# Later folded weights and a reordered start in a retention + gated-MLP kernel on one core

## The chip, the cores and the metric

The kernel runs on one core of one Trainium2 chip. The metric is the device time of one execution in microseconds (us). Before the change three runs took 1231.11, 1231.14 and 1233.21 us, a median of 1231.14 us.

## The reference, cut to what matters

```python
# q, k, v: (8, 8, 576, 64): batch, heads, positions, head size; all float32
scores = q @ k.T / sqrt(64)                      # per batch and head
ret = scores * gamma[h] ** (i - j)  (i >= j, else 0)
x = (ret @ v)  -> 4608 tokens x 512
h = max(x @ w1, x @ w2, x @ w3)                  # 512 -> 768
x = h @ w_out                                    # 768 -> 512
a = x @ u1; b = x @ u2                           # 512 -> 1024
out = ((a * b) @ u3) @ u_out                     # 1024 -> 1024 -> 512
```

Since nothing stands between `u3` and `u_out`, the kernel computes their product WC = u3 @ u_out once (the folded weights) and applies it in the last stage.

## The kernel before, in words

The program has two parts. The first, some 174 us long, is the attention with decay; the second, some 1055 us, is four stages of dense products over 12 x 384 tokens. The change touches the first part only.

**Steps.** There are 32 pairs (batch, two heads), n = 0 to 31. A loop on every engine runs over m = 0 to 16 (`STEPS` = 17). In step m the pairs `made_in(m)` = 2m, 2m+1 are begun and `read_in(m)` = 2m-2, 2m-1 are finished. TensorE (PE) does per pair: `scores(n)` (keys times queries, L1120 and L1125), `sum_state(n)` (keys times decayed values, L1140: the state that later chunks see), `query_state(n)` (L1158) and `values(n)` (L1170). VectorE (DVE) multiplies the scores by the decay (`decay_scores`, L952, `decay_tail`, L961) and chains the states (`make_state`, L974 and L977). ScalarE (ACT) makes the decayed values (`decay_values`, L793) and copies results out (`read_values`, L804 and L809). GpSimd (POOL) makes the decayed queries (`decay_queries`, L674).

**Who waits for whom.** `scores(n)` writes the PSUM banks of pair n-2 and waits for all decays of the two pairs before (`decayed`), and for `x_out` of pair n-4. `query_state(n)` waits for the states of n and for the decays of the two pairs made in the step. `decay_scores(n)` on DVE comes in its order after `make_state` of the step before. `sum_state(n)` waits for the decayed values, for the keys (`k_loaded`) and for the states of the two pairs before.

**Order inside a step on PE:** scores, then quarters of WC, then query_state, sum_state, values. For the pairs in `SUMS_FIRST` = (4, 5), that is in step 2, the sums come before query_state.

**Folded weights.** WC is made of 8 blocks kb of 4 quarters; a quarter is 6 products of 512 columns (L1185, L1187, L1189). `u3` is loaded in 8 blocks into 2 buffers, split by ACT (`split_u3`, L820) and POOL (L674) into a high and a low part; `uo` in 4 parts, split by ACT (L814) and POOL or DVE. The quarters begin in step `WC_FROM` = 3: one in step 3, three in step 4 (two of them at the step's end, `late_quarters`), two in each of the steps 5 to 14, four in steps 15 and 16.

**Start.** PE begins with products on zeros (`run_idle`, L1197), in all 9+4+3+2+2 = 20. `query_powers` and `decay_powers` (L1204, L1211) build the decay tables; `qtab` is copied by ACT (L857) after `decay_values(0)`.

**Queues.** All data is loaded by SyncE (SP), on one DMA queue, in program order: `load_qk` (queries and keys of a pair, 128 x 1152 floats, 576 KB), `load_v` and `load_k` (256 KB each), `load_tails` (64 KB), `load_decay` (128 KB), `load_uo` and `load_u3` (512 KB each). From n = 6 `load_qk(n)` waits for `q_decayed` n-3 and `load_k(n)` for `state_summed` n-1, and what stands behind such a wait in SP's order waits too.

Of the kernel before, what the change touches and what calls it, by code (L numbers as in the profile page):

```python
# [4 lines left out]
P = 128  # L5
# [5 lines left out]
FT2 = F2 // P  # L11
# [4 lines left out]
NC = SEQ // CH  # L16
# [170 lines left out]
STEPS = NP // 2 + 1  # L187
WC_FROM = 3
QUARTERS = 4 * FT2

SUMS_FIRST = (4, 5)

# [9 lines left out]
def quarters(m):  # L204
    if m == WC_FROM:
        return range(1)
    if m == WC_FROM + 1:
        return range(1, 2)
    if m >= STEPS - 2:
        return range(QUARTERS - 4 * (STEPS - m), QUARTERS - 4 * (STEPS - m) + 4)  # L210
    return range(2 * (m - WC_FROM), 2 * (m - WC_FROM) + 2) if m >= WC_FROM else ()


def late_quarters(m):
    return range(2, 4) if m == WC_FROM + 1 else ()

# [10 lines left out]
def keys_sem(n):  # L227
    return 2 + n if n < 4 else n % 2


def keys_count(n):
    return 16 if n < 4 else 16 * ((n - 4) // 2 + 1)

# [10 lines left out]

U3_LOAD = {min(2 * kb + WC_FROM - 2, STEPS - 3): kb for kb in range(FT2)}
U3_SPLIT = {min(2 * kb + WC_FROM - 1, STEPS - 2): kb for kb in range(FT2)}
UO_SPLIT = {2: 0, 3: 1}
WC_READ = {min(2 * kb + WC_FROM + 1, STEPS - FT2 + kb): kb for kb in range(FT2)}
# [18 lines left out]
def build(nc, qk, vv, vt, kk, wB, wC, wI, u3T, uo, decay, powers, columns, outT):  # L267
# [11 lines left out]
    with ctx:  # L279
# [61 lines left out]
        ks = [at(f"ks{i}", [P, K_COLS], f32, (v_at + 6 * V_COLS * 4, o)[i]) for i in range(2)]  # L341
        ks_first = [at(f"ks_first{i}", [P, K_COLS], f32, 26112 + i * K_COLS * 4) for i in range(4)]
        qks_first = [at(f"qks_first{i}", [P, KQ_COLS], f32, 34304 + i * KQ_COLS * 4) for i in range(2)]
        o += K_COLS * 4
# [24 lines left out]
        def sem(name):  # L369
            return ctx.enter_context(nc.semaphore(name))  # L370
# [5 lines left out]
        vt_loaded = [sem(f"vt_loaded{i}") for i in range(3)]  # L376
        k_loaded = [sem(f"k_loaded{i}") for i in range(6)]
        dec_loaded = [sem(f"dec_loaded{i}") for i in range(2)]
# [55 lines left out]
        def keys_of(n):  # L434
            return ks_first[n] if n < 4 else ks[n % 2]

# [8 lines left out]
        def _(sp):  # L445
# [21 lines left out]
            def load_k(n):  # L467
                if n >= 6:
                    sp.wait_ge(state_summed, n - 1)
                sp.dma_start(keys_of(n)[:, :], kk[n, :, :]).then_inc(k_loaded[keys_sem(n)], 16)  # L470
# [89 lines left out]
            sp.dma_start(pows[0:HEADS, :], powers).then_inc(pows_loaded, 16)  # L560
            sp.dma_start(cols[:, :], columns).then_inc(cols_loaded, 16)
            load_v(0)
            load_k(0)
            load_qk(1)
            load_decay(1)
            load_v(1)
            load_k(1)
            load_qk(2)
            load_qk(3)
            load_v(2)  # L570
            load_v(3)
            load_k(2)
            load_k(3)
            load_tails(0)
            load_qk(4)
# [5 lines left out]
            for m in range(1, STEPS):  # L581
                if m == 1:
                    load_u3(0)
                    load_uo(0)
                if m == 2:
                    for n in made_in(3):
                        load_k(n)
                if m > 1 and m in U3_LOAD:
                    load_u3(U3_LOAD[m])
                if m in P1_W_LOAD:  # L590
                    load_weight(P1_W_LOAD[m])
                if m >= 4:
                    for n in made_in(m + 1):
                        load_k(n)
                for n in made_in(m + 2):
                    load_qk(n)
                for n in read_in(m):
                    if n >= PAIRS:
                        store_x(n)
                if 2 * m + 4 < NP:  # L600
                    load_two_v(m + 2)
                if m == 2:
                    load_uo(2)
                    load_uo(3)
                    for n in made_in(4):
                        load_k(n)
                if m == 1:
                    load_tails(2)
                    load_uo(1)
                if 2 * m + 4 < NP:  # L610
                    load_tails(m + 2)
                if m in WC_READ:
                    store_wc(WC_READ[m])
# [58 lines left out]
        def _(pool):  # L672
# [80 lines left out]
            nc.gpsimd.memset(pows[:, :], 0.0).then_inc(pows_zeroed, 1)  # L753
            for m in range(STEPS - 1):
                if m in U3_SPLIT:
                    split_u3(U3_SPLIT[m])
                for n in made_in(m):
                    decay_queries(n)
                if m == 3:
                    split_uo(1)  # L760
                    split_uo(2)
                    split_uo(3)
                if m in P1_W_SUM:
                    sum_weight(*P1_W_SUM[m])
                if m in P1_T:
                    combine(0, P1_T[m])
# [16 lines left out]
        def _(act):  # L783
# [72 lines left out]
            act.wait_ge(qtab_powers, 1)  # L856
            nc.scalar.copy(qtab[:, :], ps[:, 2, :]).then_inc(qtab_made, 1)  # L857
            decay_values(1)
            for m in range(STEPS):
                if m == 2:  # L860
                    split_u3(U3_SPLIT[m])
                if m in UO_SPLIT:
                    split_uo(UO_SPLIT[m])
                if m in U3_SPLIT and m != 2:
                    split_u3(U3_SPLIT[m])
                if m in WC_READ and not late_quarters(m):
                    read_wc(WC_READ[m])
                for n in read_in(m):
                    read_values(n)
                if m == 3:  # L870
                    split_uo(2)
                for n in made_in(m + 1):
                    decay_values(n)
                if m == 3:
                    split_uo(3)
                if m in WC_READ and late_quarters(m):
                    read_wc(WC_READ[m])
                if m in P1_W_HI:
                    split_weight(P1_W_HI[m], 0)
                    split_weight(P1_W_HI[m], 1)  # L880
                if m in P1_HI:
                    split_tokens(0, P1_HI[m])
# [55 lines left out]
        def _(dve):  # L938
# [50 lines left out]

            def split_uo(i):  # L990
                dve.wait_ge(uo_hi, i + 1)
                low(uolo[:, 2 * i:2 * i + 2, :], uoraw[:, 2 * i:2 * i + 2, :], uohi[:, 2 * i:2 * i + 2, :]
                    ).then_inc(uo_lo[i], 1)

            def split_weight(wi, part):
# [17 lines left out]
            for m in range(STEPS):  # L1013
                for n in made_in(m):
                    decay_scores(n)
                    if n == 0:
                        mask_decay()
                        make_state(n)
                for n in made_in(m):
# [5 lines left out]
                for n in made_in(m):  # L1025
                    if n:
                        make_state(n)
                if m == 2:
                    split_uo(0)

# [76 lines left out]
        def _(pe):  # L1107
            def scores(n):
                pe.wait_ge(qk_loaded[rows_sem(n)], rows_count(n))
                if n >= 2:  # L1110
                    pe.wait_ge(decayed, 3 * (n - n % 2))
                if n == 1:
                    pe.wait_ge(qtab_made, 1)
                if n >= 4:
# [95 lines left out]
            def query_powers():  # L1210
                nc.tensor.matmul(ps[:, 2, :], pows[:, 2 * P:3 * P], pows[:, 3 * P:], start=True, stop=True,  # L1211
                                 skip_group_check=True).then_inc(qtab_powers, 1)

            pe.wait_ge(idle_zeroed, 1)
            run_idle(9, S_WC)
            pe.wait_ge(zeroed, 10)
            for m in range(STEPS):
                for n in made_in(m):
                    scores(n)
                    if n == 0:  # L1220
                        pe.wait_ge(pows_loaded, 16)
                        decay_powers()
                        query_powers()
                        run_idle(4, 3)
                        sum_state(0)
                        run_idle(3, 3)
                    if n == 1:
                        pe.wait_ge(dec_made, 1)
                        run_idle(2, S_WC)
                        pe.wait_ge(state_made, NC)  # L1230
                        sum_state(1)
                        run_idle(2, S_WC)
                for i in quarters(m):
# [4 lines left out]
                for n in read_in(m):  # L1238
                    query_state(n)
                for n in made_in(m) if m else ():  # L1240
# [4 lines left out]
                for i in late_quarters(m):  # L1245
                    wc_quarter(i)

# [115 lines left out]
```

## Time and profile before

| | |
|---|---|
| median of 3 runs | 1231.14 us |
| the profiled execution, its own time | 1231.38 us |
| its span | 1229.5 us |
| PE busy | 1222.1 us, 99% |
| DVE, ACT, POOL busy | 737.7, 485.7, 433.3 us |
| granted TensorE clock | 1.0 |
| DMA queue, share of 16 engines over the span | 39.1% |

Busy time is the time in which an instruction of the engine runs; the span goes from the first to the last instruction. With PE at 99% the time can only change by what PE executes and by where it waits. The steps of the first part can be told in the PE timeline by the two groups of `scores`.

### The profile page before, as it was taken

What the parts mean: (1) busy time and instruction counts of PE and PEld (TensorE: products, weight loads), DVE (VectorE), ACT (ScalarE), POOL (GpSimd) and SP (SyncE); (2) the same over time, 40 slices, a digit from 0 to 9 for tenths busy, and PEclk for the clock granted to TensorE, in tenths of its full rate; (3) what the DMA queues carried; (4) which work ended last, traced back from release to release, by engine and by line L of the source; (5) the groups of instructions that cost most, each with busy time, mean ns of one, the idle gap of its engine ahead of it and who ended that gap; (6) DMA issues with size and microseconds to landing.
All of it is one profiled execution on the core that took longest, in us unless ns stands there. A gap on an engine that the chain in (4) does not pass through costs nothing. (4 is left out here: it accounts for less than half of the span.)

```text
span 1229.5 us, 21665 instructions
## 1 busy us (share of the span) xinstructions
PE 1222.1 (99%) x8594; PEld 1202.2 (98%) x8594; DVE 737.7 (60%) x1065; ACT 485.7 (40%) x781; POOL 433.3 (35%) x234
## 2 busy tenths in 40 slices
PE   9999999999999999999999999999999999999999
PEld 8899999999999999999999999999999999999998
DVE  6444648845545464668886777454545466786653
ACT  3433544523232232326655544242323234554441
POOL 3535528220201102053867761202020217366550
PEclk9999999999999999999999999999999999999999
DMA  9999934121203021054464441313131342444441
GB/s 346 337 337 353 336 125 146 52 78 38 92 26 104 26 70 60 34 173 144 152 228 171 160 157 52 104 52 110 52 116 53 109 179 96 154 155 161 159 157 65
DMA packets 87332, 169.55 MB, mean 138 GB/s; under 512 B 9272, under 2 KB 58680, under 8 KB 87232
## 3 DMA queue, kind: packets, MB, share of 16 engines
q1 hardware_dynamic: 87232, 168.17, 39.1%
q8 instruction: 68, 1.11, 0.4%
q14 instruction: 32, 0.26, 0.1%
HBM read 106.27 MB, written 61.87 MB: 137 GB/s over the span
## 5 line engine op out<-in xcount | busy, mean ns | idle before, releaser
L1261 PE MATMUL ps<-chi,whi 128*128 128x384 f32 x2016 | 674.4, 335 | 1.9 <-ACT w L931 0.7
L1263 PE MATMUL ps<-chi,wlo 128*128 128x384 f32 x2016 | 673.5, 334 | 0.0
L1262 PE MATMUL ps<-clo,whi 128*128 128x384 f32 x2016 | 673.4, 334 | 0.0
L674 POOL TENSOR_TENSOR raw<-raw,raw 128x768 f32<-128x768 f32 (+3 forms) x102 | 268.1, 2650 | 582.8 <-DMA raw<-xd 203.5
L1261 PEld LDWEIGHTS ps<-chi,whi 128*128 128x128 f32 x2016 | 378.4, 188 | 4.5 <-ACT w L931 1.4
L1262 PEld LDWEIGHTS ps<-clo,whi 128*128 128x128 f32 x2016 | 378.4, 188 | 0.0
L1263 PEld LDWEIGHTS ps<-chi,wlo 128*128 128x128 f32 x2016 | 378.4, 188 | 0.0
L940 DVE TENSOR_TENSOR clo<-raw,chi 128x768 fp32r<-128x768 f32 (+2 forms) x168 | 253.5, 1537 | 41.7 <-ACT chi L851 41.7
L851 ACT CAST chi<-raw 128x768 fp32r<-128x768 f32 (+2 forms) x168 | 180.1, 1081 | 90.5 <-PE ps L1263 48.1
L931 ACT COPY w<-ps 128x384 f32<-128x384 f32 x126 | 60.5, 480 | 238.4 <-PE ps L1263 237.0
L918 ACT COPY u<-ps 128x384 f32<-128x384 f32 x126 | 60.7, 482 | 160.5 <-PE ps L1263 158.9
L1074 DVE TENSOR_TENSOR h<-ps,u 128x384 f32<-128x384 f32 x66 | 36.6, 555 | 122.8 <-PE ps L1263 121.2
L1048 DVE TENSOR_TENSOR h<-ps,w 128x384 f32<-128x384 f32 x66 | 36.6, 555 | 93.3 <-PE ps L1263 87.2
L1048 DVE TENSOR_TENSOR w<-ps,w 128x384 f32<-128x384 f32 x60 | 33.4, 557 | 87.0 <-PE ps L1263 86.9
L897 ACT COPY s<-ps 128x384 f32<-128x384 f32 x126 | 60.6, 481 | 55.5 <-PE ps L1263 55.5
L910 ACT COPY h<-ps 128x384 f32<-128x384 f32 x66 | 31.6, 479 | 82.4 <-PE ps L1263 79.8
L1074 DVE TENSOR_TENSOR u<-ps,u 128x384 f32<-128x384 f32 x60 | 33.3, 555 | 49.6 <-PE ps L1263 49.6
L674 POOL TENSOR_TENSOR wraw<-w,wraw 128x256 f32<-128x256 f32 (+2 forms) x21 | 26.2, 1247 | 95.2 <-DMA w<-wC 67.8
L940 DVE TENSOR_TENSOR wlo<-wraw,whi 128x768 fp32r<-128x768 f32 (+4 forms) x42 | 57.9, 1390 | 2.8 <-POOL wraw L674 2.7
L674 POOL TENSOR_TENSOR qdec<-qks,qtab 128x512 f32<-128x512 f32 x30 | 38.5, 1306 | 41.9 <-PE ps L1158 41.9
L952 DVE TENSOR_TENSOR probs<-ps,dec 128x512 f32<-128x512 f32 x64 | 39.9, 683 | 22.1 <-PE ps L1125 22.1
L674 POOL TENSOR_TENSOR wraw<-wraw 128x256 f32<-128x256 f32 (+2 forms) x42 | 47.4, 1129 | 1.6
(61 smaller groups left out, 820.7 us busy)
## 6 DMA issues: line engine op xcount, KB each, us to landing
gd<-h SPq DMA_DIRECT2D x96, 192.0 KB, 1.9
raw<-gd SPq DMA_DIRECT2D x24, 768.0 KB, 6.3
qks<-qk SPq DMA_DIRECT2D x30, 576.0 KB, 7.3
hd<-h SPq DMA_DIRECT2D x72, 192.0 KB, 1.9
raw<-hd SPq DMA_DIRECT2D x24, 576.0 KB, 6.6
x2d<-h SPq DMA_DIRECT2D x48, 192.0 KB, 2.9
raw<-x2d SPq DMA_DIRECT2D x24, 384.0 KB, 4.5
outT<-h SPq DMA_DIRECT2D x48, 192.0 KB, 1.9
```

The lines of the kernel that those rows point to most:

```text
L674: return nc.gpsimd.tensor_tensor(out_, a, b, op)
L851: nc.scalar.copy(chi[st][pos][:, :, :], raw_block(tau, pos)[:, :, :]).then_inc(c_hi, 1)
L897: nc.scalar.copy(sbuf_s[it % 2][:, :], ps[:, X[it % 2], 0:N]).then_inc(s_made, 1)
L918: nc.scalar.copy(sbuf_u[it % 2][:, :], ps[:, X[it % 2], 0:N]).then_inc(u_made, 1)
L931: nc.scalar.copy(sbuf_w[it % 2][:, :], ps[:, X[it % 2], 0:N]).then_inc(w_made, 1)
L940: return nc.vector.tensor_tensor(out_, whole, hi.bitcast(f32), ALU.subtract)
L952: nc.vector.tensor_tensor(probs[n % 4][:, h, 0:NC * CH].rearrange("p (n c) -> p n c", c=CH), ps[:, 2 * (n % 2) + h, :].rearrange("p (n c) ...
L1048: nc.vector.tensor_tensor(to[:, :], ps[:, Z[g % 2], 0:N], sbuf_w[g % 2][:, :], ALU.add).then_inc(sum22, 1)
L1074: nc.vector.tensor_tensor(to[:, :], ps[:, Z[g % 2], 0:N], sbuf_u[g % 2][:, :], ALU.add).then_inc(sum12, 1)
L1261: nc.tensor.matmul(to, w1, x1, start=(start and k == 0), stop=False, skip_group_check=True)
L1262: nc.tensor.matmul(to, w1, x2, start=False, stop=False, skip_group_check=True)
L1263: last = nc.tensor.matmul(to, w2, x1, start=False, stop=(k == KH[st] - 1), skip_group_check=True)
```

## The change

The folded weights start in step 5: two quarters in each of the steps 5 to 12, four (a whole block) in steps 13 to 16. `late_quarters` goes. The loads and splits of `u3` and `uo` move with them: the first `u3` is loaded in step 3 and not in step 1, `uo` in steps 1 to 4, and in steps 11 to 14 the load of `u3` stands at the end of SP's step. Two more key buffers let keys 4 and 5 have places of their own, so that keys 6 and 7 are loaded in step 1 with no wait. `SUMS_FIRST` now holds 4 to 9, so the sums come first in steps 2, 3 and 4. On PE the first two steps are written out in another order, with 13 products on zeros, and SP loads the queries and keys of pair 1 ahead of the values and keys of pair 0.

```diff
-WC_FROM = 3
+WC_FROM = 5
+WC_WHOLE = 13
-SUMS_FIRST = (4, 5)
+SUMS_FIRST = (4, 5, 6, 7, 8, 9)
 def quarters(m):
-    if m == WC_FROM:
-        return range(1)
-    if m == WC_FROM + 1:
-        return range(1, 2)
-    if m >= STEPS - 2:
+    if m >= WC_WHOLE:
         return range(QUARTERS - 4 * (STEPS - m), QUARTERS - 4 * (STEPS - m) + 4)
-def late_quarters(m):
-    return range(2, 4) if m == WC_FROM + 1 else ()
-U3_LOAD = {min(2 * kb + WC_FROM - 2, STEPS - 3): kb for kb in range(FT2)}
-U3_SPLIT = {min(2 * kb + WC_FROM - 1, STEPS - 2): kb for kb in range(FT2)}
-UO_SPLIT = {2: 0, 3: 1}
+WC_STEP = [min(2 * kb + WC_FROM, STEPS - FT2 + kb) for kb in range(FT2)]
+U3_LOAD = {WC_STEP[kb] - 2: kb for kb in range(FT2)}
+U3_SPLIT = {WC_STEP[kb] - 1: kb for kb in range(FT2)}
+UO_LOAD = {1: (0,), 2: (1,), 3: (2,), 4: (3,)}
+UO_SPLIT = {3: (0,), 4: (1,), 5: (2, 3)}
...
 # SP, the first loads
+            load_qk(1)
+            load_decay(1)
             load_v(0)
             load_k(0)
-            load_qk(1)
-            load_decay(1)
+            load_qk(2)
+            load_qk(3)
             load_v(1)
             load_k(1)
-            load_qk(2)
-            load_qk(3)
...
 # SP, the loop
                 if m == 1:
-                    load_u3(0)
-                    load_uo(0)
-                if m == 2:
-                    for n in made_in(3):
-                        load_k(n)
-                if m > 1 and m in U3_LOAD:
+                    load_k(6)
+                    load_k(7)
+                for i in UO_LOAD.get(m, ()) if m > 1 else ():
+                    load_uo(i)
+                if m in U3_LOAD and m < WC_WHOLE - 2:
                     load_u3(U3_LOAD[m])
-                if m >= 4:
+                if m >= 3:
                     for n in made_in(m + 1):
                         load_k(n)
...
                 if m == 1:
                     load_tails(2)
-                    load_uo(1)
+                    load_uo(0)
                 if 2 * m + 4 < NP:
                     load_tails(m + 2)
+                if m in U3_LOAD and m >= WC_WHOLE - 2:
+                    load_u3(U3_LOAD[m])
...
 # DVE, the states of pairs 0 and 1
-                        make_state(n)
+                        make_state(0)
+                    if n == 3:
+                        make_state(1)
...
 # PE, the start
-            run_idle(9, S_WC)
+            run_idle(8, S_WC)
             pe.wait_ge(zeroed, 10)
+            scores(0)
+            pe.wait_ge(pows_loaded, 16)
+            decay_powers()
+            query_powers()
+            scores(1)
+            pe.wait_ge(dec_made, 1)
+            run_idle(1, S_WC)
+            pe.wait_ge(qtab_made, 1)
+            sum_state(0)
+            run_idle(4, S_WC)
+            scores(2)
+            scores(3)
+            query_state(0)
+            pe.wait_ge(state_made, NC)
+            sum_state(1)
+            values(0)
+            query_state(1)
+            values(1)
+            sum_state(2)
+            sum_state(3)
+            for m in range(2, STEPS):
```

## Rows read from the trace of the kernel before

**Rows 1.** The page: PE's busy time, and DMA busy in tenths of 40 slices.
```profile
PE 1222.1 (99%) x8594; PEld 1202.2 (98%) x8594; DVE 737.7 (60%) x1065; ACT 485.7 (40%) x781; POOL 433.3 (35%) x234
DMA  9999934121203021054464441313131342444441
```
**Rows 2.** Timeline of PE, the start: start us, length us, line, records, wait before.
```profile
1.06 4.10 PE L1197 MATMUL ps<-idle 128*128 128x128 f32 x18 [1.06 <-DVE idle L1007]
...
8.20 1.05 PE L1197 MATMUL ps<-idle 128*128 128x128 f32 x8
9.19 0.69 PE L1140 MATMUL ps<-vdec,ks_first 128*64 128x64 f32 x16
...
14.01 1.16 PE L1120 MATMUL ps<-qks 64*128 64x128 f32 x16
...
16.82 0.99 PE L1158 MATMUL ps<-qdec,state 64*64 64x128 f32 x16 [0.35 <-DVE probs L952]
```
**Rows 3.** Timeline of ACT, the start.
```profile
6.37 0.91 ACT L793 ACTIVATE vdec<-vs,cols 128x256 f32<-128x256 f32 x2 [4.15 <-DMA vs<-vv]
8.40 0.59 ACT L857 COPY qtab<-ps 128x512 f32<-128x512 f32 x1 [1.13 <-PE ps L1211]
```
**Rows 4.** Timeline of DVE, the start.
```profile
9.92 0.22 DVE L974 COPY state<-ps 128x64 f32<-128x64 f32 x1 [1.51 <-PE ps L1140]
10.18 0.91 DVE L977 SCALAR_TENSOR_TENSOR state<-state,cols,ps 128x64 f32<-128x64 f32 x3
12.04 1.29 DVE L952 TENSOR_TENSOR probs<-ps,dec 128x512 f32<-128x512 f32 x2 [0.95 <-PE ps L1125]
13.36 0.50 DVE L961 TENSOR_TENSOR probs<-ps,dec 64x128 f32<-64x128 f32 x2
```
**Rows 5.** One DMA each, issue and landing: values 0, queries 1, keys 8.
```profile
L453 SPq DMA_DIRECT2D vs<-vv x1: 427/427/427, 2.5 to 2.5; - x1
DMA to landing us min/median/max: 3.9/3.9/3.9
...
L450 SPq DMA_DIRECT2D qks_first<-qk x1: 441/441/441, 3.4 to 3.4; - x1
DMA to landing us min/median/max: 5.7/5.7/5.7
...
L470 SPq DMA_DIRECT2D ks<-kk x1: 328/328/328, 35.6 to 35.6; - x1
DMA to landing us min/median/max: 7.1/7.1/7.1
```
**Rows 6.** Timeline of PE: begin of steps 2, 3, 4, 5, 6, and inside 2 and 4.
```profile
21.99 1.16 PE L1120 MATMUL ps<-qks 64*128 64x128 f32 x16
...
24.37 1.15 PE L1140 MATMUL ps<-vdec,ks 128*64 128x64 f32 x32
25.45 1.76 PE L1158 MATMUL ps<-qdec,state 64*64 64x128 f32 x32
...
29.27 1.16 PE L1120 MATMUL ps<-qks 64*128 64x128 f32 x16
...
37.98 1.16 PE L1120 MATMUL ps<-qks 64*128 64x128 f32 x16
...
40.88 0.49 PE L1120 MATMUL ps<-qks 64*128 64x128 f32 x4 [0.84 <-issue]
...
50.79 1.16 PE L1120 MATMUL ps<-qks 64*128 64x128 f32 x16
...
60.88 1.16 PE L1120 MATMUL ps<-qks 64*128 64x128 f32 x16
```
**Rows 7.** Loads of u3 (median to landing); its last split on ACT and POOL.
```profile
u3raw<-u3T SPq DMA_DIRECT2D x8, 512.0 KB, 6.6
...
154.62 1.05 ACT L820 CAST u3hi<-u3raw 128x1024 fp32r<-128x1024 f32 x1
...
155.75 2.39 POOL L674 TENSOR_TENSOR u3lo<-u3raw,u3hi 128x1024 fp32r<-128x1024 f32 x1 [3.24 <-ACT u3hi L820]
```

More of the change, by code:

```diff
@@ L227, in keys_sem @@
 def keys_sem(n):
-    return 2 + n if n < 4 else n % 2
+    return 2 + n if n < 6 else n % 2
 def keys_count(n):
-    return 16 if n < 4 else 16 * ((n - 4) // 2 + 1)
+    return 16 if n < 6 else 16 * ((n - 6) // 2 + 1)
 def v_sem(n):
@@ L342, in build @@
         ks_first = [at(f"ks_first{i}", [P, K_COLS], f32, 26112 + i * K_COLS * 4) for i in range(4)]
+        ks_first += [at(f"ks_first{i}", [P, K_COLS], f32, 36864 + i * K_COLS * 4) for i in (4, 5)]
         qks_first = [at(f"qks_first{i}", [P, KQ_COLS], f32, 34304 + i * KQ_COLS * 4) for i in range(2)]
@@ L376, in build @@
         vt_loaded = [sem(f"vt_loaded{i}") for i in range(3)]
-        k_loaded = [sem(f"k_loaded{i}") for i in range(6)]
+        k_loaded = [sem(f"k_loaded{i}") for i in range(8)]
         dec_loaded = [sem(f"dec_loaded{i}") for i in range(2)]
@@ L434, in keys_of @@
         def keys_of(n):
-            return ks_first[n] if n < 4 else ks[n % 2]
+            return ks_first[n] if n < 6 else ks[n % 2]
         def rows_of(n):
@@ L467, in load_k @@
             def load_k(n):
-                if n >= 6:
+                if n >= 8:
                     sp.wait_ge(state_summed, n - 1)
@@ L561, in _ @@
             sp.dma_start(cols[:, :], columns).then_inc(cols_loaded, 16)
+            load_qk(1)
+            load_decay(1)
             load_v(0)
             load_k(0)
-            load_qk(1)
-            load_decay(1)
+            load_qk(2)
+            load_qk(3)
             load_v(1)
             load_k(1)
-            load_qk(2)
-            load_qk(3)
+            load_tails(0)
             load_v(2)
@@ L573, in _ @@
             load_k(3)
-            load_tails(0)
             load_qk(4)
@@ L601, in _ @@
                     load_two_v(m + 2)
[L602 to L606, printed above, removed]
                 if m == 1:
                     load_tails(2)
-                    load_uo(1)
+                    load_uo(0)
                 if 2 * m + 4 < NP:
                     load_tails(m + 2)
+                if m in U3_LOAD and m >= WC_WHOLE - 2:
+                    load_u3(U3_LOAD[m])
                 if m in WC_READ:
@@ L754, in _ @@
             for m in range(STEPS - 1):
+                for i in UO_SPLIT.get(m, ()):
+                    split_uo(i)
                 if m in U3_SPLIT:
@@ L856, in _ @@
             act.wait_ge(qtab_powers, 1)
-            nc.scalar.copy(qtab[:, :], ps[:, 2, :]).then_inc(qtab_made, 1)
+            nc.scalar.copy(qtab[:, :], ps[:, S_STATE, :]).then_inc(qtab_made, 1)
             decay_values(1)
             for m in range(STEPS):
-                if m == 2:
+                for i in UO_SPLIT.get(m, ()):
+                    split_uo(i)
+                if m in U3_SPLIT:
                     split_u3(U3_SPLIT[m])
[L862 to L866, printed above, removed]
+                if m in WC_READ:
                     read_wc(WC_READ[m])
@@ L869, in _ @@
                     read_values(n)
-                if m == 3:
-                    split_uo(2)
                 for n in made_in(m + 1):
                     decay_values(n)
[L874 to L877, printed above, removed]
                 if m in P1_W_HI:
@@ L988, in mask_decay @@
                     mask.unsqueeze(1).broadcast_to([P, 4, CH]), ALU.mult).then_inc(dec_made, 1)
[L990 to L993, printed above, removed]
             def split_weight(wi, part):
@@ L1025, in _ @@
                 for n in made_in(m):
-                    if n:
+                    if n > 1:
                         make_state(n)
-                if m == 2:
-                    split_uo(0)
             merge = {B: ALU.max, I: ALU.mult}
@@ L1111, in scores @@
                     pe.wait_ge(decayed, 3 * (n - n % 2))
-                if n == 1:
-                    pe.wait_ge(qtab_made, 1)
                 if n >= 4:
@@ L1210, in query_powers @@
             def query_powers():
-                nc.tensor.matmul(ps[:, 2, :], pows[:, 2 * P:3 * P], pows[:, 3 * P:], start=True, stop=True,
+                nc.tensor.matmul(ps[:, S_STATE, :], pows[:, 2 * P:3 * P], pows[:, 3 * P:], start=True, stop=True,
                                  skip_group_check=True).then_inc(qtab_powers, 1)
             pe.wait_ge(idle_zeroed, 1)
-            run_idle(9, S_WC)
+            run_idle(8, S_WC)
             pe.wait_ge(zeroed, 10)
-            for m in range(STEPS):
+            scores(0)
[19 more added lines that the diff above has]
+            for m in range(2, STEPS):
                 for n in made_in(m):
                     scores(n)
[L1220 to L1232, printed above, removed]
                 for i in quarters(m):
@@ L1239, in _ @@
                     query_state(n)
-                for n in made_in(m) if m else ():
+                for n in made_in(m):
                     if n not in SUMS_FIRST:
@@ L1244, in _ @@
                     values(n)
-                for i in late_quarters(m):
-                    wc_quarter(i)
             def product(g, i, bank, start):
```

4 lines of the change are left out of this document (removed).

## The prediction, made before the run

> **What bounds the kernel now.** I read the page first: PE is busy for 1222.1 of 1229.5 us, and the DMA engines are at nine tenths in the first slices [rows 1]. Then the waits of PE: in the first part only one wait of size is left after the start, 0.84 us that no semaphore explains [rows 6]. So the time is PE's list of instructions plus a few us, and two questions decide: how many instructions on zeros go, and whether the pieces that moved make PE wait where it did not. Then the timelines of the first 60 us, and the landings of single DMAs.
>
> The DMA side matters more than its 39% of the span suggests. I count KB in SP's order. Queries 1 end the first 1890 KB (576+128+28+70+256+256+576) and land at 3.4+5.7 = 9.1; keys 8 end the first 13794 KB and land at 35.6+7.1 = 42.7 [rows 5]. That is 11904 KB in 33.6 us, 354 KB/us, and keys 8 took 7.1 us although their own 256 KB are worth 0.7 us at that rate: they stood behind a full queue. In this stretch a landing is set by the KB ahead of it, not by its issue.
>
> **The baseline up to step 5.** Steps begin at 21.99 (2), 29.27 (3), 37.98 (4), 50.79 (5), 60.88 (6) [rows 6]. A step without quarters takes 29.27-21.99 = 7.28, one with two 10.09: 1.40 for a quarter. Before, four quarters were done by step 5; without them it would begin at 50.79-5.60 = 45.19. The same 32 quarters are done in both kernels, and steps 5 to 16 differ in nothing but where the quarters lie, so the change is the new begin of step 5 less 45.19.
>
> **Start, steps 0 and 1.** 20 products on zeros become 13. The first nine take 4.10 for 18 records, two records a product: 0.46 each; the later ones 0.24 [rows 2]. Removed: 0.46+6x0.24 = 1.9 us. That would be the gain if nothing else were late. But the chain behind it moves:
> - Values 0 now stand behind queries 1 and decay 1. They end the first 1762 KB. They landed at 2.5+3.9 = 6.4 as KB 1058, and KB 1890 lands at 9.1 [rows 5]; between the two, 1762 KB is 8.7.
> - decay_values(0) 0.91, then the copy of qtab 0.59 [rows 3], with hand-overs of 0.05: qtab_made at 10.3. Before, this copy ended at 8.99 and was waiting for PE.
> - sum_state(0) must now wait for that: 10.4 to 11.1 (0.69 [rows 2]). PE has scores(1) and one product on zeros done by about 9.5 and waits 0.9. Keys 0 (2018 KB) land at 9.5 and do not bind.
> - DVE: make_state(0) takes from 9.92 to 11.09, 1.17; decay_scores(1) 1.29; the two tails 0.50 [rows 4]. 11.1+1.17+1.29+0.50 = 14.1. scores(2) needs all of it. Before it began at 14.01 [rows 2], so the 1.9 us are gone, as waits (the four products on zeros fill 0.95 of 3.0 us).
> - From there the old distances: query_state(0) came 2.81 behind scores(2) [rows 2], now at 16.95, ends 17.9. sum_state(1), 0.6, comes behind it and no longer ahead: 18.5. make_state(1), 1.17, follows the third and fourth decay and that sum: 19.7. values(0) (half of 29.27-25.45-1.76 [rows 6], 1.0) ends 19.5, so query_state(1) runs 19.85 to 20.8, values(1) to 21.8, sums 2 and 3 (25.45-24.37 [rows 6]) to 22.9. Step 2 begins at 22.9, before at 21.99: +0.9. Bounds: all zeros removed and no wait, 20.1 (21.99-1.9); values 0 only as late as queries 1 before, 9.1, 23.3.
>
> **Step 2.** Both states of pairs 2 and 3 now follow the last sums: DVE is at 22.9+2x1.17 = 25.2 before it takes decay_scores(4); before it was free in time. query_state(2) needs the first decay of the two, 26.5, and query_state(3) the second, 27.7. PE comes to query_state(2) at 22.9+(25.45-21.99) = 26.4 [rows 6]: two waits of about 0.2. Step 3 begins at 22.9+7.28+0.4 = 30.6 (0 to 1.0 for the waits).
>
> **Steps 3 and 4.** Both put the sums first, like step 2, with no quarter. Step 4 begins at 37.9, and reaches sum_state(8) 2.38 later (24.37-21.99 [rows 6]), 40.3. What is late there is the keys. In the new order keys 8 end the first 13346 KB and keys 9 the first 13602 KB (uo 0 to 2 and u3 0 are still ahead; uo 3, 512 KB, went behind, and 64 KB of tails came before: 13794-512+64). Taken back from the landing of KB 13794 at 42.7 by 354 KB/us: 41.4 and 42.2 [rows 5]. In the old order they were asked for after scores, quarters and query_state, near 40.88+0.6+1.4+1.76 = 44.6 [rows 6], with over 1 us to spare; that cover is gone twice, by the quarters that left and by the sums put first. PE waits 1.1 for keys 8, then 0.3 for keys 9. From the second sum to the next step it is 4.90-0.54 = 4.36 (29.27-24.37, less half the pair of sums [rows 6]), with 0.1 for hand-overs: step 5 begins at 42.2+4.36+0.1 = 46.65. Note what this does: once the keys decide, all that is won or lost before 40.3 changes nothing. Bounds of the landing: none late, step 5 at 45.2; the rate as low as 330 KB/us, 2 us later.
>
> **The 0.84 us in step 4.** The step took 12.81, with three quarters it should take 7.28+4.20 = 11.48: 1.33, 0.84 of it the wait, the rest refilling and one more group of quarters. Its cause does not show. I let it go in the sum, since PE stands at keys 8 in the same step anyway; if it comes back behind the keys, it costs 0.8 to 1.3.
>
> **What moved without a price.** The late loads of u3: that of the last block is issued behind the stores of step 14, some 3 us into step 15; 6.6 to land, 1.05 and 2.39 to split [rows 7] is 13.0, and PE asks for it when step 15 ends, 7.28+5.60 = 12.9 after its begin. 0.1 at the worst; the queue is emptier there, so nothing. The splits of uo on POOL (2.4 each) fall in steps 3 to 5 before decay_queries, whose next use is a step later. One group of quarters and the single ones go: -0.2, inside the 1.33 above. DVE loses the split of uo 0, which nothing waited for.
>
> **Sum.** 46.65-45.19 = +1.46. Profiled execution: 1231.38+1.46 = 1232.84; it stood 0.24 above the median of the runs shown, so 1232.6.
>
> **A rule weighed.** The trace shows two speeds of PE: 18 records on zeros in 4.10 us at the start, 0.23 each, and 8 in 1.05 later, 0.13, though the granted clock reads 1.0 in both [rows 2]. The Trainium skill (TensorE: Matmul & The Clock Gate, section "What's actually happening") says that the throttled state is the default and activity releases it; the start agrees. It speaks against a start with 0.9 and 2.1 us of waiting in it. The mechanism, from rows: if PE falls to the lower of its two levels (1.2 of 2.4 GHz) at scores(2) and comes back only after as long as at the start, 4.1 us of stretch hold 2.05 us of extra time; step 2 at 24.9, step 4 at 39.7, no wait for keys 8, step 5 at 47.1: +1.9, since the keys had taken 1.4 of it already.
>
> **Rivals.**
> - A, faster, 0.17: the requests of the start overlap better, values 0 land as early as 7.7, step 2 begins at 21.9, and the keys come in time. Then step 5 is at 21.9+3x7.28 = 43.7, -1.5: 1229.7. For: the rate of the first 10 us is read from two landings only. Against: 354 KB/us held over 33 us. Only with step 2 before 20.9, too, would it reach -2.5 (0.07).
> - B, slower, 0.25: the unexplained wait is one of PE's instruction stream under a full DMA queue. PE now runs steps 2 to 4 with more instructions per us and the queue as full. Place: steps 4 to 6, behind keys 9. Price 1.1, deciding from the first one not hidden by the keys: +2.6, 1233.8; two of them +3.7. For: the wait has no semaphore. Against: just one in five such steps.
> - C, the clock falls, 0.08: +1.9, 1233.0.
> - D, the change removes no wait and adds none (the keys land by 40.3, DVE keeps up), 0.12: step 5 at 22.9+21.84 = 44.7, or 45.2 with the waits of step 2: -0.5 to 0, 1231.0.
> - My forecast, the start's gain eaten and the keys deciding, 0.38: 1232.6 (1231.8 to 1233.4).
>
> **How the numbers follow.** The range takes A to B: 1229.5 to 1234.5. 0.2%, about what a measurement tells from no change, is 2.46 us: 1228.7 and 1233.6. Faster: the end of A, 0.07. Slower: B, the late end of my forecast (keys at 43.3 or later) and a bit of C, 0.27. The rest, 0.66, is the same.
>
> **What would show it.** qtab_made near 10.3 and an idle PE ahead of scores(2) (right), or sum_state(0) before 9.5 (A). Step 2 beginning near 22.9. In step 4 a wait of L1140 for the DMA of keys, 1.1 to 1.4 long; if it isn't there, my main term is wrong. Step 5 at 46.65. A wait "issue" behind it is B; records of scores(2) at double length are C. A wait of L1185 for POOL in steps 13 to 16 would make the free part wrong.

## The result: 1.2% slower, and the loss sits where the prediction saw none

The changed kernel took 1245.15 us in the median of 5 runs (1244.33 to 1250.91), the kernel before 1231.14: a ratio of 1.0121, 95% interval 1.0099 to 1.0143. I had forecast 1232.6, and a range up to 1234.5.

The profiled execution is the longest of the five: 1250.91 us, span 1249.1. These are the lines of its page that stand beside [rows 1], with the granted clock between them:

```profile
PE 1227.0 (98%) x8580; PEld 1208.6 (97%) x8580; DVE 729.9 (58%) x1064; ACT 487.7 (39%) x781; POOL 430.1 (34%) x235
PEclk9999889999999999999999999999999999999999
DMA  9999654212030202132546451213121243444441
```

PE has 14 records fewer and is busy 4.9 us longer, and the granted clock, flat before, dips in slices 5 and 6, from 125 to 187 us. The waits of PE (engine, line, what it waited for: us in total, times, longest) name the place:

```profile
PE ps L1095 <- ACT xst L799: 11.1, 3, 4.9
PE ps L1242 <- DVE wlo L922: 2.2, 1, 2.2
PE ps L1095 <- DVE probs L943: 2.0, 1, 2.0
PE ps L1115 <- issue: 1.7, 1, 1.7
```

L1095 is `scores`, L799 ACT's copy of finished values (`read_values`), L1115 `sum_state`. Here are the beginnings of steps 1, 2, 3, 4 and 5 (to be read beside [rows 2] and [rows 6]), then the first product of the second part, and last that product in the kernel before:

```profile
13.83 1.16 PE L1095 MATMUL ps<-qks 64*128 64x128 f32 x16 [2.01 <-DVE probs L943]
...
22.51 1.16 PE L1095 MATMUL ps<-qks 64*128 64x128 f32 x16
...
30.46 1.16 PE L1095 MATMUL ps<-qks 64*128 64x128 f32 x16
...
37.74 1.16 PE L1095 MATMUL ps<-qks 64*128 64x128 f32 x16
...
41.92 1.34 PE L1115 MATMUL ps<-vdec,ks 128*64 128x64 f32 x32 [1.73 <-issue]
43.19 3.25 PE L1133 MATMUL ps<-qdec,state 64*64 64x128 f32 x32
...
48.57 1.16 PE L1095 MATMUL ps<-qks 64*128 64x128 f32 x16
...
192.83 0.44 PE L1242 MATMUL ps<-chi,whi 128*128 128x384 f32 x1
```
```profile
173.90 0.44 PE L1261 MATMUL ps<-chi,whi 128*128 128x384 f32 x1
```

So 18.9 us are lost before the second part begins. The first five steps went nearly as forecast: 22.5 for 22.9, 30.5 for 30.6, 37.7 for 37.9, then the wait for the keys. Step 5 began at 48.57 and not at 46.65. The larger part of that is the clock, which fell behind the wait: the granted clock reads 0.53 from 43 to 46 us, and query_state took 3.25 us where it takes 1.76 elsewhere. The rest stands in steps 12 to 15. Here is PE at the end of step 12 (values), at the beginning of step 13, and where query_state follows the four quarters; then the same two places for steps 14 and 15:

```profile
127.23 2.15 PE L1145 MATMUL ps<-probs,vs 128*64 128x128 f32 x40
134.17 2.08 PE L1095 MATMUL ps<-qks 64*128 64x128 f32 x16 [4.78 <-ACT xst L799]
...
144.37 1.76 PE L1133 MATMUL ps<-qdec,state 64*64 64x128 f32 x32
...
150.60 1.16 PE L1095 MATMUL ps<-qks 64*128 64x128 f32 x16 [1.41 <-ACT xst L799]
...
158.66 1.76 PE L1133 MATMUL ps<-qdec,state 64*64 64x128 f32 x32
...
168.43 2.08 PE L1095 MATMUL ps<-qks 64*128 64x128 f32 x16 [4.94 <-ACT xst L799]
...
178.60 1.76 PE L1133 MATMUL ps<-qdec,state 64*64 64x128 f32 x32
```

From scores to query_state it is 8.06 in step 14, and 10.20 and 10.17 in steps 13 and 15, which follow the long waits: 16 records of scores take 2.08 us for 1.16. PE is at the lower of its two levels there (1.2 of 2.4 GHz): the granted clock reads 0.50 from 134.0 to 138.6 us. The sum: 3.38 at step 5 (48.57 less 45.19), waits 4.78+1.41+4.94 = 11.13, slow clock 2.14+2.11 = 4.25: 18.8 of 18.9.

The next rows show what ACT did ahead of the first of these copies, what POOL did, and what SP had issued:

```profile
131.95 1.04 ACT L810 CAST u3hi<-u3raw 128x1024 fp32r<-128x1024 f32 x1 [7.77 <-DMA u3raw<-u3T]
132.90 0.58 ACT L816 COPY wcst<-ps 128x512 f32<-128x512 f32 x1
133.38 1.18 ACT L799 COPY xst<-ps 128x576 f32<-128x576 f32 x2
```
```profile
133.07 2.35 POOL L666 TENSOR_TENSOR u3lo<-u3raw,u3hi 128x1024 fp32r<-128x1024 f32 x1 [11.79 <-ACT u3hi L810]
135.37 2.52 POOL L666 TENSOR_TENSOR qdec<-qks,qtab 128x512 f32<-128x512 f32 x2
```
```profile
119.03 3.98 SPq L479 DMA_DIRECT2D xd<-xst  x4
...
124.34 0.66 SPq L485 DMA_DIRECT2D u3raw<-u3T  x1
126.98 0.80 SPq L466 DMA_DIRECT2D ks<-kk  x2
136.73 1.56 SPq L446 DMA_DIRECT2D qks<-qk  x2
...
142.33 0.59 SPq L485 DMA_DIRECT2D u3raw<-u3T  x1
```

Read together, they give a chain. Step 12 begins at 119.24. The load of u3 block 4, now at the end of SP's step 11 behind four stores and the loads of values and tails, is issued at 124.34 and lands 7.6 us later. ACT stands at split_u3 for 7.77 us, and behind it in ACT's order wait read_wc and read_values. PE has ended values(22) and values(23) by 129.4, and scores(26) waits for ACT's copy of pair 22. That is the first wait. Then POOL: decay_queries(24) stands behind POOL's half of the same split and comes at 135.37. SP's load of queries 28 waits for it and is issued at 136.73, ten us behind the keys. The stores and the next u3 stand behind that load, and this u3 is issued at 142.33. So one late load makes the next one late, and PE's wait comes again in each step.

### The profile page after: what moved, and what is told of

Same layout as the page of the kernel before. It is cut to its first block, busy times and chain, and to the rows that moved or that the text cites. A ratio compares the mean times of both kernels' runs of the same rounds, so it can differ in the third digit from the quotient of the medians.

```text
span 1249.1 us, 21640 instructions
## 1 busy us (share of the span) xinstructions
PE 1227.0 (98%) x8580; PEld 1208.6 (97%) x8580; DVE 729.9 (58%) x1064; ACT 487.7 (39%) x781; POOL 430.1 (34%) x235
## 4 chain that ended last, share of the span: by engine, by line
PE 95%; issue 2%; DVE 1%; DMA 1%; POOL 1%; SPq 0%; ACT 0%; ACTq 0%; DVEq 0%; POOLq 0%
PE ps L1242 28%; PE ps L1244 28%; PE ps L1243 28%; PE ps L1095 2%; PE ps L1145 2%; PE ps L1133 2%; PE ps L1160 1%; DMA u3raw<-u3T 1%; PE ps L1115 1%; PE ps L1162 1%; PE ps L1164 1%; PE ps L1100 0%; DVE probs L934 0%; POOL qdec L666 0%; PE ps L1172 0%
## 5 line engine op out<-in xcount | busy, mean ns | idle before, releaser
L922 DVE TENSOR_TENSOR clo<-raw,chi 128x768 fp32r<-128x768 f32 (+2 forms) x168 | 244.0, 1480 | 25.8 <-ACT chi L841 25.8
L1095 PE MATMUL ps<-qks 64*128 64x128 f32 x480 | 37.9, 302 | 13.2 <-ACT xst L799 11.1
L666 POOL TENSOR_TENSOR qdec<-qks,qtab 128x512 f32<-128x512 f32 x30 | 37.7, 1277 | 35.1 <-PE ps L1133 35.1
```

The lines of the kernel that those rows point to most:

```text
L666: return nc.gpsimd.tensor_tensor(out_, a, b, op)
L922: return nc.vector.tensor_tensor(out_, whole, hi.bitcast(f32), ALU.subtract)
L1095: nc.tensor.matmul(ps[:, 2 * (n % 2) + h, c * CH:(c + 1) * CH], rows_of(n)[own, keys:keys + CH], rows_of(n)[own, c * CH:(c + 1) * CH], sta ...
```

## The experiments

Each kernel ran on the same chip as the kernel before (whose medians there are 1231.17 to 1231.81), and the ratios are to that. **Theory 1** is the chain above. **Rivals**: whole blocks in steps 13 and 14 are too much in themselves; the clock falls of itself; the new start is at fault.

**x1, the changed kernel again.** No edit.

> The changed kernel once more, as the control beside the edits. Its first profile was of its longest execution (1250.91 us; the others 1244.3 to 1248.1). Expected 1244 to 1246 us against 1231.1 of before, with three waits of PE for ACT's copy of the values at the ends of steps 12, 13 and 14 (4.78, 1.41, 4.94 us in the first profile) and the wait ahead of sum_state(8) in step 4 (1.73). If the stretches at the lower TensorE clock vary from execution to execution, the places of the waits stay and only the stretches behind them change.

1245.38 us, ratio 1.0108 (1.0085 to 1.0131). The profiled execution, 1245.60 us, is a usual one. The waits for L799 are 9.1 us in three. The clock stayed up in step 4, and step 5 began at 46.62, where I had forecast 46.65:

```profile
41.56 1.32 PE L1115 MATMUL ps<-vdec,ks 128*64 128x64 f32 x32 [1.05 <-issue]
42.81 1.76 PE L1133 MATMUL ps<-qdec,state 64*64 64x128 f32 x32
...
46.62 1.16 PE L1095 MATMUL ps<-qks 64*128 64x128 f32 x16
```

**x2, the late loads moved ahead of the stores.**

```diff
+                if m in U3_LOAD and m >= WC_WHOLE - 2:
+                    load_u3(U3_LOAD[m])
                 for n in read_in(m):
                     if n >= PAIRS:
                         store_x(n)
...
-                if m in U3_LOAD and m >= WC_WHOLE - 2:
-                    load_u3(U3_LOAD[m])
```

> The changed kernel, with the loads of u3 in steps 11 to 14 taken from the end of SP's step to a place between the loads of queries and the stores of results. Theory 1 (the late load: ACT stands at split_u3 for a DMA that was issued behind the stores, and read_values, for which PE's next scores wait, is queued behind it): the three waits of PE at the ends of steps 12 to 14 go, 11.1 us and the slow stretches behind them; 1233.5 to 1236 us remain, 2 to 4 above before, from the first five steps. Rival 2 (whole blocks in steps 13 and 14 are themselves too much for an engine, or the DMA is simply full there): the time stays above 1240. Rival 3 (the clock falls of itself): the clock stays at or below 0.996 in the mean.

1240.27 us, ratio 1.0073 (1.0058 to 1.0088): 5 us back, where I expected 10. It is above the 1240 that I had given to rival 2, so the time alone does not put that rival out; x7 does. Two of the three waits are gone, one of 4.41 is left at the end of step 13. ACT's own rows give another reason for it:

```profile
141.31 1.04 ACT L810 CAST u3hi<-u3raw 128x1024 fp32r<-128x1024 f32 x1 [8.18 <-DMA u3raw<-u3T]
145.19 0.58 ACT L816 COPY wcst<-ps 128x512 f32<-128x512 f32 x1 [2.83 <-DMA wcd<-wcst]
145.67 1.19 ACT L799 COPY xst<-ps 128x576 f32<-128x576 f32 x2
```

With a whole block in each step read_wc runs in steps 12, 13, 14, one after the other, and the staging buffer for WC must have been stored in between; that store, too, is issued at the end of SP's step. My theory was incomplete: a second thing on ACT waits for the end of SP's list.

**x3, one load alone.** `load_u3` of block 4 back at the head of SP's step 11.

```diff
-                if m in U3_LOAD and m < WC_WHOLE - 2:
+                if m in U3_LOAD and m < WC_WHOLE - 1:
...
-                if m in U3_LOAD and m >= WC_WHOLE - 2:
+                if m in U3_LOAD and m >= WC_WHOLE - 1:
```

> The changed kernel, with one load moved: that of u3 block 4 (step 11) stands at the beginning of SP's step again; those of blocks 5 to 7 stay at the end. Theory 1 with the loop (ACT late, POOL's decay_queries late, SP's load of queries late, the next u3 late): the first wait (4.8 us and the slow clock behind it) goes and the two others, which it set off, shrink to 0 to 1.5 us each; 1235 to 1238 us. If each late load made its wait by itself and not through the one before, the waits at steps 13 and 14 stay at 1.4 and 4.9 us: 1238 to 1241.

1238.71 us, ratio 1.0065 (1.0047 to 1.0082). That is above the range for the loop (1235 to 1238) and inside the one for waits made one by one (1238 to 1241). The first wait went, the second fell to 0.18, the third stayed, 4.19, so by itself this run does not decide between the two. Its rows show the chain begin one block later: the split of block 5 on ACT at 138.39, the decayed queries on POOL at 141.83, SP's load of queries at 143.18, the next u3 at 149.11. One load of eight was worth 6.7 us against x1.

**x7, all of it.** As x3, and from step 12 on the u3 loads, and in all steps the stores of WC, ahead of the stores of results.

```diff
-                if m in U3_LOAD and m < WC_WHOLE - 2:
+                if m in U3_LOAD and m < WC_WHOLE - 1:
...
+                if m in U3_LOAD and m >= WC_WHOLE - 1:
+                    load_u3(U3_LOAD[m])
+                if m in WC_READ:
+                    store_wc(WC_READ[m])
                 for n in read_in(m):
                     if n >= PAIRS:
                         store_x(n)
...
-                if m in U3_LOAD and m >= WC_WHOLE - 2:
-                    load_u3(U3_LOAD[m])
-                if m in WC_READ:
-                    store_wc(WC_READ[m])
```

> The changed kernel with the load of u3 block 4 at the beginning of SP's step 11 and, from step 12 on, the loads of u3 and in all steps the stores of WC between the loads of queries and the stores of results. Moving the loads alone left one wait of 4.4 us in step 13, where ACT's read_wc stood for a store of WC that SP had issued at the end of its step. If that and the late loads are the whole cause, no wait for ACT's copies is left at the ends of steps 12 to 14, the clock reads 0.999 or more, and the time is that of the first five steps: +1.5 to +2.5, 1232.7 to 1233.7. If whole blocks in steps 13 and 14 cost by themselves: above 1236.

1233.03 us, ratio 1.0010 (1.0001 to 1.0020). PE has no wait of any kind between 100 and 175 us (the mean granted clock is 0.998 in this profile, 0.001 under my forecast for it, since it fell at the start). The quarters still come four to a step in steps 13 to 16: no step of PE waits for whole blocks, and that rival is out. What remains, +0.1 to +2.5 by the interval, holds what I had forecast for the whole change (+1.46). Its waits:

```profile
PE ps L1095 <- DVE probs L943: 2.0, 1, 2.0
PE ps L1115 <- issue: 1.8, 1, 1.8
```

The agreement is one of totals. In the profiled execution the second part began 3.65 us later than before, and then took 2.0 us less, although no edit touches it:

```profile
177.55 0.44 PE L1242 MATMUL ps<-chi,whi 128*128 128x384 f32 x1
```

Over all 14 profiles the second part took 1053.4 to 1056.3 us. So a difference of one or two us between two profiled executions says nothing of an edit unless its wait is seen.

**x8, and keys 8 and 9 first.**

```diff
+                if m == 3:
+                    load_k(8)
+                    load_k(9)
                 for i in UO_LOAD.get(m, ()) if m > 1 else ():
                     load_uo(i)
...
-                if m >= 3:
+                if m >= 4:
                     for n in made_in(m + 1):
                         load_k(n)
```

> As x7, and keys 8 and 9 are loaded at the beginning of SP's step 3, ahead of uo 2 and u3 0 (1024 KB, 2.9 us at 354 KB/us). The wait of 1.1 to 1.7 us ahead of sum_state(8) goes, step 5 begins at 45.2 to 45.5; 1.2 to 1.7 us less than x7, 1231.3 to 1232.3. If queries 10 and 11, which come behind, are late instead: no gain.

1232.15 us, ratio 1.0003 (0.9994 to 1.0013). The wait ahead of sum_state(8) is gone and step 5 begins at 45.50: keys 8 landed at 39.3, for 41.5 in x1. Against x7 the time is 0.9 less by the medians (expected 1.2 to 1.7), within what the two intervals leave open. The trace decides here, since it shows the wait itself:

```profile
40.60 1.15 PE L1118 MATMUL ps<-vdec,ks 128*64 128x64 f32 x32
41.69 1.76 PE L1136 MATMUL ps<-qdec,state 64*64 64x128 f32 x32
...
45.50 1.16 PE L1098 MATMUL ps<-qks 64*128 64x128 f32 x16
```

Part of the gain is given back at once: in step 5 PE waits 0.78 us for DVE's decayed scores, and the step takes 11.09 us for 10.09.

**x4, the sums of step 4 behind query_state.** `SUMS_FIRST = (4, 5, 6, 7)`.

> The changed kernel with SUMS_FIRST = (4, 5, 6, 7): in step 4 query_state comes before sum_state again, which gives the keys 8 and 9 some 1.7 us more. Theory 1: the wait of 1.7 us ahead of sum_state(8) falls to below 0.5, and with it the slow clock in the query products behind it; step 5 begins at 45.5 to 46.5 and not at 48.6; 2 to 3 us less than the control: 1242 to 1243.5. If the keys do not decide: no change within 0.5 us. It also tells whether a gain in step 4 is kept to the end, given the waits in steps 12 to 14.

1246.86 us, ratio 1.0118 (1.0098 to 1.0138): no gain, a miss. In its profile step 4 did what I expected, from 39.45 to 47.44 in 7.99 us where the first profile of the changed kernel took 10.83, with no wait for keys. But the clock had fallen in step 1, which made step 2 begin 1.4 us later than in x1, so step 5 came 0.8 later than in x1 all the same; and the waits for L799 were 10.8, for 9.1 there. Whether a gain in step 4 is kept to the end, this pair cannot say.

**x5, the new start on the kernel before**, and **x6, the old start on the changed kernel.** The edits are those of the diff at the head that belong to steps 0 and 1 (SP's first loads, the written-out order of PE, `make_state(1)`, `query_powers`), made alone and undone alone.

> The kernel before with the change's first two steps alone: the new order on PE, the new order of SP's first loads, state 1 after the fourth decay, 13 products on zeros for 20. Everything from the loop on, the folded weights included, is as before. From the traces so far: step 2 begins at 22.5 to 22.8 and not at 21.99, and two waits of 0.2 follow in step 2; +0.8 to +1.3 us, 1232.0 to 1232.5. If the start were what costs most of the 14 us, some 1240. If its removed products pay: 1230.

> The changed kernel with the old first two steps (20 products on zeros, old orders of PE, SP and DVE there); the folded weights from step 5 on, the sums first in steps 2 to 4, and the late loads as changed. If the start hardly matters, since the keys in step 4 and the late u3 decide: within 1.5 us of the control, 1243.5 to 1246. The waits at the ends of steps 12 to 14 stay at 9 to 11 us.

x5: 1231.08 us in 10 runs, ratio 0.9993 (0.9982 to 1.0005). x6: 1247.41, 1.0127 (1.0106 to 1.0147), with waits for L799 of 8.5 us. Both times lie outside what I expected, x5 by 0.9 us below and x6 by 1.4 above. Still, the start is innocent of the 14 us, and its cost, +0.9 by my working, can't be told from nothing by time.

**x9, ACT copies the values out before it splits u3** (from step 12 on), SP untouched.

```diff
-                if m in U3_SPLIT:
+                if m in U3_SPLIT and m < WC_WHOLE - 1:
                     split_u3(U3_SPLIT[m])
                 if m in WC_READ:
                     read_wc(WC_READ[m])
                 for n in read_in(m):
                     read_values(n)
+                if m in U3_SPLIT and m >= WC_WHOLE - 1:
+                    split_u3(U3_SPLIT[m])
```

> The changed kernel, nothing moved on SP: from step 12 on ACT copies the values out (read_values) before it splits u3 (split_u3) and not behind it. If ACT's order is what carries the late load to PE, the three waits of PE for ACT's copies at the ends of steps 12 to 14 go, at the price of quarters of WC that may come late in steps 13 to 16 (u3_lo is later by the copies, some 2 to 4 us after the landing): 1233 to 1238 us. If the late load reaches PE on another way (queries or values that land late, because SP is late), the waits stay in another form and the time above 1240.

1259.44 us, ratio 1.0218 (1.0201 to 1.0234). A miss: worse by 14 us. The first wait did go, as the theory has it (scores(26) at 129.77, right behind values):

```profile
129.77 1.16 PE L1097 MATMUL ps<-qks 64*128 64x128 f32 x16
...
152.59 2.08 PE L1097 MATMUL ps<-qks 64*128 64x128 f32 x16 [5.44 <-ACT xst L799]
```
```profile
151.32 0.59 ACT L816 COPY wcst<-ps 128x512 f32<-128x512 f32 x1 [16.44 <-DMA wcd<-wcst]
```

But PE then stood for u3_lo (2.82 us in step 13 and 4.10 in step 16), and ACT for 16.44 us at read_wc, for the store of WC that SP had issued at 143.67, behind queries that waited for POOL, which waited for the split. The waits at the ends of steps 13 and 14 came back longer, 5.44 and 5.93. The order on ACT decides which instruction shows the wait; the lateness is SP's.

**x10, POOL makes the decayed queries before it splits u3** (from step 12 on).

```diff
-                if m in U3_SPLIT:
+                if m in U3_SPLIT and m < WC_WHOLE - 1:
                     split_u3(U3_SPLIT[m])
                 for n in made_in(m):
                     decay_queries(n)
+                if m in U3_SPLIT and m >= WC_WHOLE - 1:
+                    split_u3(U3_SPLIT[m])
```

> The changed kernel, nothing moved on SP or ACT: from step 12 on POOL makes the decayed queries of a step before it splits u3. That cuts the loop in which a late u3 makes decay_queries late, that SP's next load of queries (it waits for q_decayed), and that the next u3 behind it. The first wait (end of step 12, 3.2 to 4.8 us) is made by the first late load and stays; if the loop exists, the second goes (1.4 to 1.9 before) and the third (4.0 to 4.9) falls below 1: 1238 to 1241 us. If there is no loop: 1244 to 1246.

1241.92 us, ratio 1.0086 (1.0072 to 1.0100), 0.9 above my range. The waits are as expected: the first stays, the second is gone, the third falls to 0.50; a small one for POOL is new:

```profile
132.04 2.08 PE L1097 MATMUL ps<-qks 64*128 64x128 f32 x16 [4.21 <-ACT xst L801]
...
160.69 1.16 PE L1097 MATMUL ps<-qks 64*128 64x128 f32 x16 [0.50 <-ACT xst L801]
...
174.74 0.50 PE L1162 MATMUL ps<-uohi,u3hi 128*128 128x512 f32 x1 [1.20 <-POOL u3lo L666]
```

SP's load of queries 28, which the first profile has at 136.73, no longer waits for the split:

```profile
126.34 0.85 SPq L446 DMA_DIRECT2D qks<-qk  x2
```

That shows the loop over POOL and SP.

**x11 and x12, a faster version?** x11 is the kernel before with 12 products on zeros for 20. x12 has the start of x11 and the loop of x8. The edit of x11:

```diff
-            run_idle(9, S_WC)
+            run_idle(8, S_WC)
...
-                        run_idle(4, 3)
+                        run_idle(1, 3)
                         sum_state(0)
-                        run_idle(3, 3)
+                        run_idle(2, 3)
...
-                        run_idle(2, S_WC)
+                        run_idle(1, S_WC)
                         pe.wait_ge(state_made, NC)
                         sum_state(1)
-                        run_idle(2, S_WC)
```

> The kernel before with 12 products on zeros for 20 (8, 1, 2, 1, 0 at its five places) and nothing else changed. In the old order the copy of qtab waits for PE and not for a load, so they are on the path: scores(2) at 12.4 and not at 14.01. Queries 4 and 5 and keys 4 and 5 land at 19 to 23.7 whatever PE does, so 0.8 to 1.6 us are left: 1229.6 to 1230.4 by 1231.2 to 1231.8 for before, if the clock rises as early as with 9 products at the start. If the zeros only filled waits: no change.

> The folded weights from step 5 as in the change, with the loads and stores of WC placed as in x8 (u3 4 early, the later ones and WC's stores before the stores of results, keys 8 and 9 first in step 3), and the old first two steps with 12 products on zeros. If the start in its old order is the better one and the late part is free: step 2 at 20.5 to 21.5, 1230 to 1231.5. If the DMA decides the first five steps, as the forecast had it, x12 stands within 0.5 us of x8 (1232.15).

x11: 1230.83 us, 0.9995 (0.9987 to 1.0004). x12: 1230.07, 0.9993 (0.9984 to 1.0001). Neither beats the kernel before beyond its interval. In x11 step 2 begins at 21.00, one us earlier, and PE then waits for ACT's vdec (0.96 in step 4) and for ACT's read_wc at a quarter (0.89 in step 5): in its profile all is given back, and the second part begins at 174.54. x12 reads the lowest median, 1.5 us under before, and its interval ends at 1.0001. Its profile does not show where that would come from: the second part begins when it did before (173.90), and only that part, which no edit touches, is shorter:

```profile
173.96 0.44 PE L1236 MATMUL ps<-chi,whi 128*128 128x384 f32 x1
```

## Why the prediction was wrong, by its own steps

**Start, steps 0 and 1: right in mechanism and size.** The 1.9 us of removed zeros turned into a wait of 2.01 us ahead of scores(2). Forecast 14.1, measured 13.83; step 2 forecast at 22.9, measured at 22.51. sum_state(0) ran at 10.05, forecast 10.4; the wait of 0.9 that I had put ahead of it was not there in this profile, while x4 and x7 have 0.65 and 0.42.

**Step 2: right.** Step 3 began 7.95 later (forecast 7.7), with the second wait of 0.21 and sums some 0.15 late.

**Steps 3 and 4: right in the wait and its cause, too strong in the rule.** Keys 8 landed at 33.6+8.2 = 41.8 (forecast 41.4) and sum_state(8) ran at 41.92; x1 put step 5 at 46.62 against 46.65, and x8, which changed against x7 only the KB ahead of the keys, took the wait away. But I had also said that the landing does not depend on the issue, and that what is lost before 40.3 then changes nothing. In x4, x7 and x9 step 2 began 1.3 to 2.2 us later than in the first profile, SP issued keys 8 at 35.0 to 35.8 (33.6 in the first profile, 33.9 in x1), and they landed at 43.3 to 43.7; in x10, 0.9 late at step 2, they landed at 41.7. SP's loads of queries wait for PE's scores and POOL's decays, so a late start can make the keys late too: step 5 of x7 began at 48.43, +3.24 and not +1.46.

**The 0.84 us in step 4** did not come back in the changed kernel as such; waits named "issue" of 0.2 to 0.6 inside groups of small products stand in x1, x6, x7, x11 and x12. The wait for the keys, too, is booked as "issue" in the profile, so the word alone tells nothing. Their cause stays open.

**"What moved without a price": this step failed, and it is nearly the whole error.** I had written that the late loads of u3 cost "0.1 at the worst; the queue is emptier there, so nothing". They cost 15.4 us in the first profile: 11.1 of waits for ACT's copies and 4.3 of slow clock behind them. I had taken steps 5 to 16 to differ in nothing but where the quarters lie; the loads lie elsewhere too. The step was wrong three times:
- I worked out the last block only, in the longest step (12.9 us) with an emptying queue. The decisive one was block 4: its step 12 is 10.1 long and the queue full (DMA share 0.94 from 119 to 124 us). My own numbers give it away: issue some 3 us into the step (measured 5.1), 6.6 to land, 1.05 to split, so 10.7, with PE asking for what ACT copies next at about 9.
- I asked when PE needs the quarters of the block. But PE's next scores wait for read_values, and read_values stands behind split_u3 in ACT's order. For each wait that an edit makes later, one must name what is queued behind it; I did so for the keys and not here. The sign that I had named for this step, PE waiting for POOL at a quarter in steps 13 to 16, does not occur in the changed kernel: I had watched the wrong place.
- I took a late load for a single delay. x10 shows a loop, ACT to POOL to SP and back, and the rows of x3 and x9 agree with it; x2 and x9 show the store of WC as a second line into it.

x7 is the proof by undoing: with these loads and stores placed elsewhere and all else as changed, the waits are gone and the ratio is 1.0010. That 1231.14+1.46 would be 1.0012 is in part luck: in x7's profile the first five steps cost 3.24 and not 1.46.

**The rivals.** A and D did not come. B (an unexplained wait behind the keys) came small: in x1 and x7 a wait of 0.29 named "issue" stands in step 5, where I had put it, and the step took 10.74 and 10.75 us for 10.09; the first profile has none. C, the clock, I gave 0.08, and it was no rare case. It fell at scores(2) in five of the ten profiles with the new start (x4, x5, x7, x9 and x10): there the 16 records of scores(3) take 2.01 to 2.08 us for 1.14, and step 2 begins at 23.42 to 24.66 for 22.51 to 22.99 in the others. It fell as well behind waits of 4 to 5 us in every profile that has them. In the first profile it made 4.25 of the 18.9 us, and some 1.5 more in step 4; I had put its price at 1.9 and looked for it in one place only. It follows a wait: with the late waits and the new start gone (x12), the mean granted clock is 1.0. The Trainium skill (TensorE: Matmul & The Clock Gate, section "What's actually happening") has activity as what lifts the throttle, and the trace agrees. In x7 the granted clock reads 0.67 from 16 to 20 us, behind the wait at scores(2) and with PE busy for 1.99 of 4 us; it is back at 1.00 after a stretch in which PE was busy throughout:

```profile
12.00:16.00 4.00, 1.99 (x28) 2.02 (x30) 2.45 (x7) 1.81 (x4) 0.82 (x1) 0.90 1.07 379
16.00:20.00 4.00, 4.00 (x60) 3.81 (x59) 2.29 (x6) 0.31 (x1) 0.87 (x1) 0.67 1.02 398
20.00:24.00 4.00, 3.71 (x84) 3.44 (x80) 1.27 (x6) 2.27 (x7) 1.67 (x2) 1.00 1.06 364
```

(The columns are: stretch, us, busy and instructions of PE, PEld, DVE, ACT, POOL, then the granted clock, DMA share, GB/s.)

## What to carry to other kernels

A load moved to the end of a queue's step is late by all that this queue waits for on the way, and its price is paid by whatever stands behind its reader in an engine's order, here long before the data itself was used. Where a load repeats, check every instance, and first the one in the shortest step and with the fullest queue. And where engines feed one another in a ring (ACT splits, POOL decays, SP waits for POOL and loads for ACT), a slip does not die out by itself: one load of eight placed earlier brought back 6.7 of 14 us.

## What the runs showed that I had not expected

- A wait of 4 to 5 us of PE costs half as much again: steps 13 and 15 of the changed kernel each took 2.1 us more at the lower clock.
- Where the wait stays near 2 us, whether the clock falls varies from execution to execution: scores(2) came behind the same 2.0 us in x1 and in x4, and PE was at full clock in the one and fell to half in the other. In the runs without the late waits the mean granted clock is below 1.0 in 15 of 30 with the new start (x5, x7, x8) and in 3 of 75 with an old one (x11, x12 and the kernel before beside them). The medians do not show it as a cost: x5 reads 0.7 us below the kernel before, within its interval.
